# Constant matmuls between the first rows, the last keys in parts of 128, and first scores in two parts, in an attention and two-network kernel on one core

## What is computed

```python
kv_pool = kv.reshape(B, H // 4, 4, W // 4, 4, C).mean(axis=(2, 4))
k = v = kv_pool.reshape(B, -1, C) @ w_sr          # 768 keys of 128 numbers an image
a = softmax(q @ k.T / sqrt(C))
x = (a @ v).reshape(B * N, C)
h = x @ w_in;   x = (h * cos(h)) @ w_out          # 128 -> 2048 -> 128
h = x @ w2_in;  x = (h * sigmoid(1.702 * h)) @ w2_out
```

## Time and profile before

| | us |
|---|---|
| median of 3 runs | 2683.49 (2683.06 to 2683.57) |
| profiled execution, its time | 2683.63 |
| profiled execution, its span | 2681.9 |
| PE busy in the span | 2658.3 |
| PE busy in the first 40 us | 28.45 |
| PE busy in the other 2641.9 us | 2629.88 |

### The profile page before, as it was taken

How to read it: one execution, slowest core, us unless ns; L and a number is a source line. 1 busy time by engine, 2 the same in 40 slices (tenths; PEclk the granted TensorE clock), 3 DMA queues, 4 the chain that set the end, 5 groups by cost and what they waited for, 6 DMA issues and landing times.

```text
span 2681.9 us, 42560 instructions
## 1 busy us (share of the span) xinstructions
PE 2658.3 (99%) x13346; PEld 2254.1 (84%) x13346; DVE 2098.5 (78%) x2772; ACT 1919.0 (72%) x2497; POOL 2028.8 (76%) x1904
## 2 busy tenths in 40 slices
PE   8999999999999999999999999999999999999999
PEld 7999999977888888888888888888888888888887
DVE  7888888877777777777777777777777777777775
ACT  4777777777777777777777777777777777777776
POOL 3887677568787878777777778787778777777773
PEclk9999999999999999999999999999999999999999
DMA  7323222200000000000000000000000000000000
GB/s 201 71 47 84 67 48 47 57 20 5 16 16 8 16 8 16 8 16 8 16 8 16 8 16 14 9 16 8 16 8 16 8 16 8 16 8 16 12 9 12
DMA packets 219124, 67.65 MB, mean 25 GB/s; under 512 B 202448, under 2 KB 203088, under 8 KB 218192
## 3 DMA queue, kind: packets, MB, share of 16 engines
q1 hardware_dynamic: 218032, 67.07, 10.9%
q10 hardware_dynamic: 1056, 0.13, 0.0%
HBM read 42.01 MB, written 25.17 MB: 25 GB/s over the span
## 4 chain that ended last, share of the span: by engine, by line
PE 97%; DVE 1%; POOL 1%; ACT 1%; DMA 0%; issue 0%; SPq 0%; POOLq 0%
PE psum L569 31%; PE psum L570 31%; PE psum L571 31%; PE psum L709 5%; POOL g_lo L554 0%; PE psum L668 0%; DMA kv_all<-in_kv 0%; ACT g_hi L906 0%; ACT turns L856 0%; DVE probs_t_lo L1009 0%; PE psum L630 0%; DVE neg_max L993 0%; POOL g_hi L551 0%; DVE g L1088 0%; DVE x_lo L1016 0%
## 5 line engine op out<-in xcount | busy, mean ns | idle before, releaser
L554 POOL TENSOR_TENSOR g_lo<-g,g_hi 128x512 fp32r<-128x512 f32 x768 | 1123.2, 1463 | 67.6 <-ACT g_hi L906 7.2
L1097 DVE TENSOR_TENSOR g_lo<-g,g_hi 128x1024 fp32r<-128x1024 f32 (+1 forms) x396 | 599.5, 1514 | 430.6 <-ACT g L901 425.3
L551 POOL CAST g_hi<-g 128x512 fp32r<-128x512 f32 x754 | 533.2, 707 | 359.9 <-DVE g L1088 359.9
L899 ACT ACTIVATE g_hi<-psum 128x1024 fp32r<-128x1024 f32 (+1 forms) x396 | 398.0, 1005 | 435.4 <-PE psum L571 435.4
L569 PE MATMUL psum<-g_hi,w_lo 128*128 128x512 f32 x1536 | 599.5, 390 | 6.1 <-POOL g_lo L554 5.5
L569 PE MATMUL psum<-x_hi,w_lo 128*128 128x512 f32 x1536 | 601.7, 392 | 0.9 <-ACT g L901 0.7
L571 PE MATMUL psum<-x_hi,w_hi 128*128 128x512 f32 x1536 | 598.1, 389 | 0.0
L570 PE MATMUL psum<-x_lo,w_hi 128*128 128x512 f32 x1536 | 598.0, 389 | 0.0
L570 PE MATMUL psum<-g_lo,w_hi 128*128 128x512 f32 x1536 | 597.6, 389 | 0.0
L571 PE MATMUL psum<-g_hi,w_hi 128*128 128x512 f32 x1536 | 597.6, 389 | 0.0
L1088 DVE TENSOR_TENSOR g<-psum,g 128x512 f32<-128x512 f32 x768 | 490.5, 678 | 5.8 <-ACT g L892 5.8
(11 more groups left out here) (78 smaller groups left out, 3037.6 us busy)
## 6 DMA issues: line engine op xcount, KB each, us to landing
x_dram<-x_out SPq DMA_DIRECT2D x48, 256.0 KB, 2.3
x_raw<-x_dram SPq DMA_DIRECT2D x48, 256.0 KB, 2.8
out<-y_blocks SPq DMA_DIRECT2D x190, 64.0 KB, 2.3
q_blocks<-in_q SPq DMA_DIRECT2D x188, 64.0 KB, 2.2
kv_all<-in_kv SPq DMA_DIRECT2D x4, 1536.0 KB, 11.5
kv_all<-in_kv SPq DMA_DIRECT2D x5, 1024.0 KB, 8.9
w_raw<-in_moe_w_in SPq DMA_DIRECT2D x2, 1024.0 KB, 7.2
kv_all<-in_kv SPq DMA_DIRECT2D x2, 512.0 KB, 14.8
```

The lines of the kernel that those rows point to most:

```text
L551: nc.gpsimd.tensor_copy(g1_hi[p % 4][:, t], g1[p % 4][:, t]).then_inc(g1_hi_ready, 1)
L554: nc.gpsimd.tensor_tensor(g1_lo[p % 4][:, t], g1[p % 4][:, t], g1_hi[p % 4][:, t].bitcast(F32), ALU.subtract).then_inc(g1_lo_ready, 1)
L899: nc.scalar.activation(g2_hi[p % 2][:, t], h2[buffer2(j)][:, t], ACT.Silu, scale=GELU)
L1097: nc.vector.tensor_tensor(g2_lo[p % 2][:, t], g2[p % 2][:, t], g2_hi[p % 2][:, t].bitcast(F32), ALU.subtract).then_inc(g2_lo_ready, 1)
```

## The change

Three things are done in the head, on top of each other.

1. **Constant matmuls.** DVE fills the first 512 columns of `w_hi` (which hold nothing until much later) with ones. PE runs matmuls of 128 x 512 on them, whose result nobody reads, at fixed places of its queue: 14 at the start, 7 after the first row piece, 2 after the second, 5 and 2 after the third and fourth, and 4 after the last projection of values. They write banks 2 and 6.
2. **The last 256 keys as two parts of 128.** `KEY_PARTS` is 256, 256, 128, 128. The last half tile is one load of 1 MB in place of two of 512 KB. DVE sums three of its four windows only, two and then one (`ROW_SUMS`). The fourth window isn't summed by DVE: PE multiplies its four tokens with `row_mean` one by one and adds up in PSUM (`pool_rows` with `rows=4`), ahead of the others, as soon as the load has landed.
3. **Order.** The scores of the first two blocks are made in two parts: the first 512 keys, then the last 256, with the projection of the last 128 keys between. The values are projected and split part by part behind the keys of the same part, but for the last part, whose projection stands behind the scores. On ACT the rounding of the last values (`round_values(3)`) stands ahead of the first exponentials, on DVE their split stands behind both maxima and ahead of the first inverse. `transpose_queries` comes before the second inverse.

The third load of image 1's kv waits for `rows_pooled` 4 in place of 3, the same point, since the counter has four steps now.

```diff
-    ROW_PIECES[-1:] = [(HT - 1, HALF_W, HALF_W // 2), (HT - 1, HALF_W + HALF_W // 2, HALF_W // 2)]
+    ROW_SUMS = [(k, w, n) for k, (t, w, n) in enumerate(ROW_PIECES[:-1])]
+    ROW_SUMS += [(len(ROW_PIECES) - 1, HALF_W, HALF_W // 2),
+                 (len(ROW_PIECES) - 1, HALF_W + HALF_W // 2, R)]
+    KEY_PARTS = [(0, TKEYS), (TKEYS, TKEYS), (2 * TKEYS, P), (2 * TKEYS + P, P)]
+    POOL_BANKS, KEY_BANKS, VALUE_BANKS = [0, 1, 6, 2], [3, 4, 5, 6], [7, 7, 4, 7]
...
+            def pool_rows(t, m, rows=1):
+
+                at = t * TKEYS + m * (P // R)
+                n = max(n for n, part in enumerate(KEY_PARTS) if part[0] <= at)
+                at -= KEY_PARTS[n][0]
+                for r in range(rows):
+                    last = nc.tensor.matmul(pool_ps[n][:, at:at + P // R], kv_tiles[t][:, m, r],
+                                            row_mean[:, :], start=r == 0, stop=r == rows - 1)
+                return last
+
+            def pool_sums(k, mark=False):
+
+                pe.wait_ge(rows_summed, k + 1)
+                piece, w, n = ROW_SUMS[k]
+                for m in range(w // R, (w + n) // R):
+                    last = pool_rows(ROW_PIECES[piece][0], m)
+                if mark:
+                    last.then_inc(rows_pooled, 1)
+
+            def keep_warm(n, ps):
+
+                for _ in range(n):
+                    nc.tensor.matmul(ps, w_hi[:, 0:P], w_hi[:, 0:TOK], start=True, stop=True)
...
+            pe.wait_ge(warm_made, 1)
+            keep_warm(14, warm_ps)
             transpose_first()
             pe.wait_ge(row_mean_made, 3)
...
+            pool_sums(0)
+            keep_warm(7, warm_ps)
+            pool_sums(1, True)
+            keep_warm(2, warm_ps)
+            pe.wait_ge(w_sr_loaded, 16)
+            project_keys(0)
             pe.wait_ge(q_lo_ready, 1)
-            pe.wait_ge(k0_split, HT)
-            score(0, 0, 0, 0)
-            score(0, 1, 1, 0)
-            for t in range(HT):
-                project_values(t)
+            project_values(0)
+            pool_sums(2)
+            keep_warm(5, warm_ps)
+            pool_sums(3, True)
+            keep_warm(2, warm_ps)
+            project_keys(1)
+            pe.wait_ge(v0_split, 1)
+            project_values(1)
+            pool_sums(4, True)
+            pe.wait_ge(rows_loaded[-1], 16)
+            pool_rows(HT - 1, WB - 1, R)
+            project_keys(2)
+            pe.wait_ge(k0_split, 2)
+            project_values(2)
+            pool_sums(5)
+            pool_sums(6, True)
+            score(0, 0, 0, 0, [0])
+            project_keys(3)
+            score(0, 1, 1, 0, [0])
+            pe.wait_ge(k0_split, 4)
+            score(0, 0, 0, 0, [BANK])
+            score(0, 1, 1, 0, [BANK])
+            pe.wait_ge(v0_split, 2)
+            project_values(3)
+            keep_warm(4, warm_late_ps)
...
             split_queries(0, 0, q_first_ps)
-            copy_tile(0)
...
+            for n in range(3):
+                copy_tile(n)
+                round_keys(n)
+                round_values(n)
+            copy_tile(3)
+            round_keys(3)
+            round_values(3)
             exponentials(0, 0, 0)
-            round_values(0)
             exponentials(1, 1, 1)
...
+            nc.vector.memset(w_hi[:, 0:TOK].bitcast(F32), 1.0).then_inc(warm_made, 1)
...
             maximum(0, 0, 0)
             maximum(1, 1, 1)
+            split_values(3)
             invert_total(0, 0)
-            split_values(0)
+            transpose_queries(1, 1)
             invert_total(1, 1)
-            split_values(1)
-            split_values(2)
-            transpose_queries(1, 1)
```

More of the change, by code:

```diff
@@ L213, in attention_and_networks, with part_of @@
     x1_ps = banks(7, TOK)
[L215 to L218, removed]
+    def part_of(bank, n):
+        return banks(bank, KEY_PARTS[n][1])
+    pool_ps = [part_of(bank, n) for n, bank in enumerate(POOL_BANKS)]
+    k_ps = [part_of(bank, n) for n, bank in enumerate(KEY_BANKS)]
+    v_ps = [part_of(bank, n).rearrange("p (t c) -> p t c", c=C)
+            for n, bank in enumerate(VALUE_BANKS)]
+    q_first_ps = banks(7, TOK)
+    warm_ps = banks(2, TOK)
+    warm_late_ps = banks(6, TOK)
     h1 = [banks(0, PAIR), banks(2, PAIR), banks(4, PAIR)]
@@ L596, in key_piece, with score @@
                 last.then_inc(piece_made, 1)
-            def score(b, j, n_s, n_q):
-                for a in range(0, KEYS, BANK):
+            def score(b, j, n_s, n_q, parts=range(0, KEYS, BANK)):
+                for a in parts:
                     z = min(a + BANK, KEYS)
@@ L624, in transpose_first, with project_keys, project_values @@
                 last.then_inc(q_transposed, 1)
[L626 to L630, removed]
+            def project_keys(n):
+                pe.wait_ge(tile_copied, n + 1)
+                at, width = KEY_PARTS[n]
+                nc.tensor.matmul(k_ps[n], w_sr_sb[:, :], pooled_t[:, at:at + width],
                                  start=True, stop=True).then_inc(k0_made, 1)
[L633 to L637, removed]
+            def project_values(n):
+                at, width = KEY_PARTS[n]
+                for m in range(width // P):
+                    last = nc.tensor.matmul(v_ps[n][:, m, :],
                                             pooled_t[:, at + m * P:at + (m + 1) * P],
@@ L1018, in split_x1 @@
                                         ALU.subtract).then_inc(x1_split, 1)
-            for k in range(2):
-                sum_rows(k)
+            sum_rows(0)
+            sum_rows(1)
             split_queries(0, 0, q_first_ps)
-            for k in range(2, 4):
-                sum_rows(k)
+            sum_rows(2)
             split_keys(0)
-            for k in range(4, len(ROW_PIECES)):
-                sum_rows(k)
+            sum_rows(3)
+            split_values(0)
+            sum_rows(4)
             split_keys(1)
+            sum_rows(5)
+            sum_rows(6)
             split_keys(2)
+            split_values(1)
+            split_values(2)
+            split_keys(3)
             def invert_total(s, j):
```

76 lines of the change are left out of this document (31 added, 45 removed).

## The result

| | before | changed |
|---|---|---|
| median | 2683.45 (20 runs) | 2678.80 (20 runs) |
| lowest to highest | 2682.79 to 2683.63 | 2678.49 to 2680.39 |
| profiled execution | 2683.63 | 2678.81 |

The changed kernel is 4.65 us faster, a ratio of 0.9984 with a 95% interval of 0.9978 to 0.9989.

A forecast was written before the change was run, and what follows sets the result against it. The prediction took PE's work plus idle time to bound the kernel, with the gain in the head: 3.1 + 0.7 + 0.4 = 4.2 us off 2683.49 gave 2679.3 us, range 2678.4 to 2682.3.

The forecast's parts named there:

- What bounds it: PE's work plus idle time; what brings PE's loop forward at 38 us comes off the end one for one.
- The clock is the lever: Constant matmuls in the head raise PE from 1.2 to 2.4 GHz; their own cost is nothing, their worth the clock.
- The prediction's sum: Head savings of 3.1 to the first maximum, 0.7 to POOL and 0.4 to PE's transposes: 4.2 us.
- Unit prices: Per matmul 0.42 or 0.23 by clock; 32-column record 0.21 or 0.11; 128-column work 0.29 on DVE, 0.28 on ACT.
- The burst: Fourteen constant matmuls at the start, 5.9 us, expected to raise the clock in or at their end, by 5.7 us worked before.
- The landing: Last rows land at 20.67 as before, one 1 MB load; 0.5 earlier or later moves the time as much.
- The range: 2678.6 to 2681.0 for the forecast's own case by other unit prices and landing; 8-in-10 range 2678.4 to 2682.3.
- main case: The forecast itself: the clock rises early and stays up, the head is 4.2 us shorter, 2679.3 us; chance 0.62.
- From scores to the loop: Behind the first maximum: POOL 0.7 more by the earlier second score, PE's transposes 0.4 more as values are split.
- The clock falls again: PE's clock drops between last constant matmul (17.7) and scores (22.75): 2681.3 to 2683.1; chance 0.24 together with late rises.
- late rises: Clock rises after the first burst with a gain left, 2.8 if at 16.5; chance 0.24 together with the falling clock.
- Slower: Clock doesn't rise in the first burst, constants hold PE up: some 6.5 us slower, 2690; chance 0.06.

The follow-up runs named there:

- late-queries: Changed kernel with the second chunk's query loads, and all behind them in SP's queue, held until the last rows have landed; median 2678.51 us.
- no last four: Changed kernel without the four constant matmuls behind the last projection of values; median 2679.15 us.
- two-load: Changed kernel with the last half tile loaded as two loads of 512 KB in place of one of 1 MB; median 2680.30 us.
- burst only: Changed kernel with the first 14 constant matmuls kept and the other 20 left out; median 2685.13 us.
- no constants: Changed kernel without any of its 34 constant matmuls, order, parts of 128 and split scores kept; median 2685.47 us.
- no burst: Changed kernel without the first 14 constant matmuls, the other 20 kept; median 2680.38 us.

## Why the prediction was right, and where it was off

- *What bounds it.* Right. The gain is all in the head, and comes off the end one for one: PE's wait of 38.25 moved to 33.50, 4.75 us, the profiled time by 4.82.
- *The clock is the lever.* Right, and more so than I had it. Without constants the change loses 2.2 us, so the constants are worth 6.7 us in the new order, 0.6 in the old one with its waits, and, with nine more, about 3.8 there in an execution that held the clock. The rest of the change is worth about 1 us at the upper clock and less than nothing at the lower. The prediction's sum gave shares to the steps without saying that they hang together.
- *Unit prices.* 0.11 for a 32-column record at the upper clock, by the six transposes: measured 0.11. DVE's and ACT's 128-column work: 0.29 and 0.28, as estimated.
- *The burst.* The rise came near its end in the profile after, at 6.60, during the twelfth of the fourteen. In the late-queries profile the same burst lasted 5.04 in place of 5.81, and the clock's record has the rise at 4.91, 1.7 us sooner, during the eighth; with no last four it came at 6.94, during the thirteenth. So the 5.7 us that PE had worked before the rise in the trace of before were no measure of it, and that the burst was long enough by them was in part luck. The margin was as thin as said in some executions and wide in others; no execution of the changed kernel shows a missed rise.
- *The landing.* This term was mis-sized: I had 20.67, it was 20.00. From there every step lies 0.45 to 0.7 ahead of the forecast: last sums 21.81 (22.5), second score parts 23.96 (24.6), maximum 24.62 (25.15), POOL 27.07 (27.65), transposes 28.69 (29.15). That is the 0.5 us between 2679.3 and 2678.8. The merged load has its share in it. With the queries behind it, the last landing of two loads was at 20.65, 20.44, 20.39 and 19.62 in four profiles, that of one load at 19.63 to 19.98 in five; executions differ by more than the cut moves it. With the queries held back the two are apart: 19.82 for two loads (one profile), 19.16 to 19.23 for one (three). So "by the same bytes in the same order" was the step that mis-sized the landing, in part; the rest is the scatter between executions.
- *The range.* The stated 2678.6 to 2681.0 of the main case don't follow from its terms: 1.2 and 0.4 us of price and 0.5 of landing around 2679.3 give 2678.8 to 2681.4 when they all add up. The measured 2678.80 lies on that lower end, by the landing.
- *From scores to the loop.* Right within 0.1: 0.77 for the second maximum, where 0.7 was forecast, and 0.32 for the values' splits, where it was 0.4. PE's transposes wait for POOL alone now.
- *The clock falls again.* It had 0.24 with late rises. Four of 20 executions lie 1.2 to 1.6 us high, and the two-load profile shows the mechanism. One reading beside it was wrong, that PE never waits 0.8 us at the upper clock and 0.55 is its longest wait there. That is so in the head only: the trace of before does show PE waiting 0.8 us at the upper clock, four times between 581 and 612 us (0.79 to 0.83), and the clock stays up, with 512-column matmuls 0.23 apart behind each wait. That spoke against the rival:

```profile
611.51 0.50 PE L569 MATMUL psum<-g_hi,w_lo 128*128 128x512 f32 x1 [0.83 <-POOL g_lo L554]
```

- *What makes it fall.* In the two-load kernel the longest wait ahead of the fall was 0.73 us, and with no last four the clock stayed up through one of 1.50. So the length of one wait doesn't tell whether the clock falls; what does isn't separated by these runs. The Trainium skill's statement on waits between bursts ("TensorE: Matmul & The Clock Gate", the part on oscillation) is borne out in its direction only: its example is of matmuls that wait for DMA between the bursts for far longer than 0.73 us. The Trainium skill's other statement, that the number of matmuls at the slow clock differs from run to run ("TensorE: Matmul & The Clock Gate", Part 1), is borne out: of the same fourteen constants seven ran at it from end to end in the late-queries profile and twelve in that of no last four.
- *Slower.* The mechanism is real: burst only and no constants are 1.9 and 2.2 us slower than before, by PE that comes late to the last rows. But they don't have the constants in the way, as the rival did. The nearest to it are the four slower executions of no burst, which have the other twenty and came to 2684.62 to 2684.87, 1.3 to 1.6 us slower than before, where the rival had 6.5 for no rise at all. In the changed kernel the case didn't occur, so its price is not shown.

## What to carry to other kernels

A change that gives TensorE more work to do early and one that keeps its clock up can each be worthless and together be worth 4.7 us: price the steps at both clock levels, and read the level from the distance between matmuls. Where the engine's work comes in spurts under a load, constant matmuls belong into the gaps up to the work that matters; here a burst at the start alone was worth 0.3 us by the medians. Then look for what shortens the waits themselves: holding back loads that weren't urgent cost one line, and no execution with it was 1.4 us high, where four of 20 had been.

## What was not expected of the hardware

- The clock fell while TensorE was at work: in the two-load kernel it ran pooling, small projections and the first scores without a wait from 20.43 on, and the clock fell at about 23.0. And it didn't rise while TensorE was busy for 4.14 of 5 us with pooling and projections (burst only, 15 to 20 us).
- The profile's granted clock reads 1.00 from the start until the clock has risen for the first time, though the matmuls are 0.42 apart (before, 26.52 to 26.94); after a fall it reads 0.50 (burst only, 15 to 20 us).
- Four loads of 64 KB in small pieces, queued behind the row loads, delayed the last of these by 0.8 us (20.0 against 19.2, and 20.65 against 19.82 in the old order).
